# Attention on one Trainium2 core: a second chunk of keys weighted in fp16 halves in place of fp32, its high half split on ScalarE and its low half on GpSimd

## The reference, cut to what matters

```python
q_n, k_n = (rmsnorm(q, g_q), rmsnorm(k, g_k))
scores = scale * np.matmul(q_n, k_n.transpose(0, 1, 3, 2))
scores = scores - np.max(scores, axis=-1, keepdims=True)
attn = np.exp(scores)
attn = attn / (np.sum(attn, axis=-1, keepdims=True) + 1e-09)
return np.matmul(attn, v).astype(np.float32)
```

## Time and profile before

| what | us |
|---|---|
| median of three runs | 1143.07 |
| the profiled execution | 1139.88 |
| its span, first to last instruction | 1138.1 |
| TensorE busy | 1100.3 (97%) |
| VectorE busy | 594.7 (52%) |
| ScalarE busy | 425.9 (37%) |
| GpSimd busy | 256.5 (23%) |
| attention, up to the first matmul of the next layer | 300.5 |
| first scores of step 0 | at 19.4 |
| steps 7 to 21, each | 11.33 |

### The profile page before, as it was taken

How to read it: one execution, slowest core, us unless ns; L and a number is a source line. 1 busy time by engine, 2 the same in 40 slices (tenths; PEclk the granted TensorE clock), 3 DMA queues, 4 the chain that set the end, 5 groups by cost and what they waited for, 6 DMA issues and landing times.

```text
span 1138.1 us, 17823 instructions
## 1 busy us (share of the span) xinstructions
PE 1100.3 (97%) x6617; PEld 573.3 (50%) x6618; DVE 594.7 (52%) x837; ACT 425.9 (37%) x631; POOL 256.5 (23%) x235
## 2 busy tenths in 40 slices
PE   7989999999999999999999999999898999999996
PEld 3434444444455555555555555556454555555554
DVE  7888888887433443333343300015656565556721
ACT  5768777777511111211111200001535253353510
POOL 4756767672200000000000000000211122112211
PEclk9999999999999999999999999999899999999999
DMA  5412222210121111111100501000848355366400
GB/s 144 122 49 62 61 65 58 66 25 17 60 67 56 56 55 55 55 55 55 55 28 1 195 28 41 28 32 23 296 163 319 118 211 206 108 217 225 142 20 18
DMA packets 71978, 104.11 MB, mean 91 GB/s; under 512 B 29310, under 2 KB 47870, under 8 KB 71920
## 3 DMA queue, kind: packets, MB, share of 16 engines
q1 hardware_dynamic: 63680, 89.84, 24.0%
q0 software_dynamic: 3120, 11.02, 2.7%
q10 hardware_dynamic: 5120, 2.48, 0.8%
HBM read 93.88 MB, written 13.76 MB: 95 GB/s over the span
## 4 chain that ended last, share of the span: by engine, by line
PE 87%; ACT 4%; DVE 4%; issue 2%; DMA 2%; ACTq 0%; POOL 0%; DVEq 0%; POOLq 0%; SPq 0%
PE ps L1434 29%; PE ps L1449 15%; PE ps L1528 12%; PE ps L1357 10%; PE ps L1506 7%; PE ps L1336 5%; PE ps L1316 2%; ACT arena L815 2%; DVE arena L1042 2%; PE ps L1348 2%; PE ps L1299 2%; PE ps L1338 1%; DMA arena<-in_moe_w 1%; PE ps L1515 1%; PE ps L1493 1%
## 5 line engine op out<-in xcount | busy, mean ns | idle before, releaser
L1434 PE MATMUL ps<-arena 128*128 128x448 f16 x1728 | 328.8, 352 | 0.0
L1434 PEld LDWEIGHTS ps<-arena 128*128 128x128 f16 x1728 | 168.1, 98 | 155.7
L1449 PE MATMUL ps<-arena 128*128 128x392 f16 (+1 forms) x1008 | 167.3, 329 | 2.4 <-DVE arena L1022 2.4
L1506 PE MATMUL ps<-arena 128*128 128x512 f16 x648 | 150.5, 388 | 5.6 <-DVE arena L1229 5.6
L1042 DVE SCALAR_TENSOR_TENSOR arena<-arena 128x768 f16<-128x768 f32 (+1 forms) x112 | 113.1, 1066 | 74.1 <-ACT arena L815 74.0
L1528 PE MATMUL ps<-arena 128*128 128x384 f16 x864 | 143.3, 326 | 4.0 <-DVE arena L1234 3.6
L1449 PEld LDWEIGHTS ps<-arena 128*128 (+1 forms) x1008 | 98.4, 98 | 70.4 <-DVE arena L1022 2.8
L1357 PE MATMUL ps<-arena 128*128 128x448 f32 x288 | 133.0, 573 | 0.0
L785 ACT ACTIVATE arena<-ps 128x448 f32<-128x448 f32 x48 | 26.1, 543 | 263.0 <-PE ps L1434 263.0
L1016 DVE SCALAR_TENSOR_TENSOR arena<-ps,arena 128x448 f32<-128x448 f32 x48 | 30.0, 624 | 176.0 <-PE ps L1434 96.1
L1528 PEld LDWEIGHTS ps<-arena 128*128 128x128 f16 x864 | 83.5, 98 | 58.6 <-issue 2.5
(11 more groups left out here) (170 smaller groups left out, 1078.7 us busy)
## 6 DMA issues: line engine op xcount, KB each, us to landing
arena<-in_moe_w SPq DMA_DIRECT2D x48, 512.0 KB, 6.3
arena<-in_moe_w SPq DMA_DIRECT2D x64, 384.0 KB, 3.9
arena<-in_qk SPq DMA_DIRECT2D x23, 448.0 KB, 3.5
y_parts<-arena SPq DMA_DIRECT2D x16, 384.0 KB, 2.3
arena<-in_v SPq DMA_DIRECT2D x48, 96.0 KB, 2.6
arena<-in_moe_w_out SPq DMA_DIRECT2D x12, 384.0 KB, 5.5
arena<-in_w_out_t SPq DMA_DIRECT2D x11, 384.0 KB, 3.1
arena<-in_moe_w_gate SPq DMA_DIRECT2D x10, 384.0 KB, 4.2
```

Of the source, the lines that this page charges most:

```text
L1434: last = nc.tensor.matmul(ps[:, 2 * (b % 2) + g, 0:S], up_w[s][:, g, c, wl], xt[:, b * KC + c, xl], start=(c == 0 and wl + xl == 0), stop= ...
L1449: last = nc.tensor.matmul(ps[:, 4 + 2 * s + h, 0:cols], gt[:, f, gl, bass.ds(t * 128, 128)], wo[:, f, wl, h, 0:cols], start=(f == 0 and gl ...
L1506: last = nc.tensor.matmul(ps[:, b, :], x_t[:, xl, c], w1_s[s][:, c, wl, b * 512:(b + 1) * 512], start=(c == 0 and xl + wl == 0), stop=(c = ...
```

## The change

The first of the three chunks of 128 keys is weighted in fp16 halves too. `exps(n, 1)` takes the smaller bias (the factor 256), so that the result fits fp16. ScalarE gets `first_high(n)` (a copy of 128x896 to fp16, after `exps(n, 2)`) and a copy of V's first chunk with its ones (128x192) in `v_high`. VectorE gets the low half of V's chunk in `v_low`, ahead of that of the last keys. GpSimd gets `first_low(n)` (128x896, probabilities less their high half) as the last item of its step. TensorE's `weigh` of chunk 0 becomes `weigh_first`: three fp16 matmuls of 128x448 for each head. There are two buffers of each new tile and four new semaphores; ScalarE also waits at the start until GpSimd has written the ones.

```diff
+        p_first = [at2.take(128, 2 * 2 * S, F16).rearrange("p (l h s) -> p l h s", l=2, h=2) for _ in range(2)]
+        v_first = [at2.take(128, 2 * 3 * D, F16).rearrange("p (l c) -> p l c", l=2) for _ in range(2)]
...
+            def first_low(n):
+
+                pool.wait_ge(p1_hi_ready, n + 1)
+                nc.gpsimd.tensor_tensor(p_first[n % 2][:, 1], probs[n % 2][:, :, 0], p_first[n % 2][:, 0], ALU.subtract)\
+                    .then_inc(p1_lo_ready, 1)
+
             for n in range(3):
                 normalise(n)
...
                 if has(n - 2):
                     x_low(n - 2)
+                if has(n):
+                    first_low(n)
...
-                    nc.scalar.activation(probs[n % 2][:, :, i - 1], ps_pair(SCORE_SLOT, 128), ACT.Exp, bias=lift[:, 1:2])\
+                    nc.scalar.activation(probs[n % 2][:, :, i - 1], ps_pair(SCORE_SLOT, 128), ACT.Exp,
+                                         bias=lift[:, 0:1] if i == 1 else lift[:, 1:2])\
                         .then_inc(probs_ready, 1)
...
+            def first_high(n):
+
+                act.wait_ge(probs_ready, 4 * n + 2)
+                nc.scalar.activation(p_first[n % 2][:, 0], probs[n % 2][:, :, 0], ACT.Copy).then_inc(p1_hi_ready, 1)
+
             def v_high(n):
 
                 act.wait_ge(v_loaded[n % 3], 64 * (n // 3) + 64)
+                nc.scalar.activation(v_first[n % 2][:, 0], v_ones[n % 3][:, 0], ACT.Copy, scale=S_OP).then_inc(v1_hi_ready, 1)
                 nc.scalar.activation(v_parts[n % 2][:, 0], v_end[n % 3], ACT.Copy, scale=S_OP).then_inc(v_hi_ready, 1)
...
             act.wait_ge(lift_ready, 2)
+            act.wait_ge(ones_ready, 3)
             act.wait_ge(scratch_ready, 1)
...
                 if has(n):
                     exps(n, 2)
+                    first_high(n)
                 if has(n - 2):
                     x_high(n - 2)
...
             def v_low(n):
 
+                dve.wait_ge(v1_hi_ready, n + 1)
+                nc.vector.scalar_tensor_tensor(v_first[n % 2][:, 1], v_ones[n % 3][:, 0], S_OP, v_first[n % 2][:, 0], ALU.mult, ALU.subtract)\
+                    .then_inc(v1_lo_ready, 1)
                 dve.wait_ge(v_hi_ready, n + 1)
...
+            def weigh_first(n, h):
+
+                pe.wait_ge(v1_lo_ready, n + 1)
+                pe.wait_ge(p1_lo_ready, n + 1)
+                for pl, vl in PASSES:
+                    nc.tensor.matmul(ps[:, 6 + h, SQ], v_first[n % 2][:, vl, h * D:h * D + 2 * D], p_first[n % 2][:, pl, h],
+                                     start=False, stop=False)
+
             def weigh(n, h, cs):
 
-                if h == 0 and cs[0] == 0:
+                if h == 0:
...
                     weigh_end(n - 1)
-                    weigh(n - 1, 0, (0,))
+                    weigh_first(n - 1, 0)
...
-                    weigh(n - 1, 1, (0,))
+                    weigh_first(n - 1, 1)
```

More of the change, by code:

```diff
@@ L278, in attention_moe_moe_kernel @@
         p_lo_ready = sem("p_lo_ready")
+        p1_hi_ready = sem("p1_hi_ready")
+        p1_lo_ready = sem("p1_lo_ready")
+        v1_hi_ready = sem("v1_hi_ready")
+        v1_lo_ready = sem("v1_lo_ready")
         v_hi_ready = sem("v_hi_ready")
```

## The result

The changed kernel takes 1155.93 us (median of four runs, 1153.12 to 1156.45) against 1142.9 of the kernel before: 1.0111 times the time, 95% interval 1.0089 to 1.0134, that is 13.0 us more. The forecast was 1158.6, in a range of 1148 to 1166, and slower with a chance of 0.87. The profiled execution took 1153.12 us, its span 1151.4, against 1139.88 and 1138.1 before.

What follows compares the result with a forecast made beforehand. TensorE was taken to bound the step, by 0.3 us over ScalarE. Fifteen steady steps at +0.76 us (+11.4) and the uneven steps summed to +15.5: 1143.07 + 15.5 = 1158.6 us, 8 in 10 within 1148 to 1166.

Steps and rivals of the forecast that it cites:

- The mechanism: Each steady attention step: VectorE's low half of V stands some 1.2 us until GpSimd's first_low ends, delaying everything behind it.
- step 4: Uneven attention step: 1.7 us gained as GpSimd's multiplication no longer blocks the low halves, 1.0 lost on ScalarE, -0.7 us together.
- TensorE's saving: Three fp16 passes for each fp32 matmul of the first chunk: up to 0.6 us less TensorE time a step.
- ScalarE's loop: The steady step if ScalarE alone set it, with its two new copies: 11.33 us, no gain, no loss.
- the sum of 12.09 us: Steady step as a loop through ScalarE, GpSimd, VectorE and back to exps: 12.09 us against 11.33, +0.76 a step.
- Step 0: First attention step: scores(1, 0) already waits for ScalarE's exps, so all new ScalarE work shows, +1.1 us.
- Step 6: Attention step with turned_high ahead on ScalarE, no longer covered: +1.1 us.
- Steps 3 and 5: Two attention steps taken to lose like the steady ones: +1.5 us together.
- Steps 1 and 2: Early attention steps, paced by ScalarE's DMA issues: no change, 0 us.
- No blocking: Rival for the steady steps: first_low releases the port early, 0 to 0.1 us a step, 1143 to 1147 us; chance 0.13.
- TensorE's saving comes through: Rival: ScalarE's copies stay hidden in its idle time, 24 x 0.6 = 14 us go, 1129 us; chance 0.05.
- The clock falls in the steady steps: Rival: new TensorE gaps lower the granted clock in each step, 1158.6 + 20 = 1179 us; chance 0.06.

Runs made afterwards that it cites:

- experiments 1: The changed kernel with two neighbours on ScalarE swapped, x_high(n-2) ahead of first_high(n): 1150.65 us against 1144.55 of the kernel before, 1.0054 times.
- experiment 2: The changed kernel without GpSimd's first_low, TensorE's third pass reading the high half again: 1149.58 us against 1144.55 of the kernel before, 1.0041 times.
- experiment 7: The changed kernel with GpSimd's first_low run twice, the second waiting for the first: 1199.93 us in one execution.
- experiment 4: The changed kernel with all four splits left out and the three fp16 passes reading constant tiles: 1134.24 us against 1144.55 of the kernel before, 0.9902 times.
- the repeated profile: The changed kernel run again, nothing altered: 1156.04 us against 1143.46 of the kernel before, 1.0101 times.
- experiment 3: The changed kernel with x_high ahead of first_high and both v_high copies moved behind end_high(n): 1137.94 us against 1144.55 of the kernel before, 0.9945 times.
- experiment 8: The changed kernel with x_high ahead of first_high and a second 128x896 copy behind first_high into a spare tile: 1171.35 us in one execution.

## Why the prediction was right, and where it was off

**The mechanism** of the steady step was right in each link, and shown by experiments 1, 2 and 7: taking the overlap away by order alone, or by leaving the GpSimd instruction out, gives back the same 0.35 us; doubling it adds 1.69. The Trainium skill's page "SBUF — State Buffer", section "SBUF: two separate sides", has the rule that the port pair which the two engines share is held for a whole instruction; the traces agree for the subtractions (1.36 us for L977 in the changed kernel, 1.97 for L984 in experiment 7). The exception seen before the change, the `pow` of 16 columns, stayed one: the two low halves took 0.35 and 0.28 us under it in step 4 of the changed kernel.

**TensorE's saving** was forecast at up to 0.6 us a step and measured alone at 0.55 (experiment 4). **ScalarE's loop** was forecast at 11.33 and measured at 11.40 (experiments 1 and 2). Without GpSimd's part the change is still a loss of some 5 us (experiment 2), but only 1.0 of it lies in steps 7 to 21 (170.95 us against 169.97); the rest is in the uneven ones, where the granted clock fell too (0.77 in step 1, 0.81 in step 4). The saving is eaten at `scores(n+1, 0)`, as written.

**The step that failed** is the size of the loop, the sum of 12.09 us, which measured 11.75. The other links were right to 0.02 us each. Off were:

- `first_low`: 1.89 us and not 2.0. I took a value near twice the 448-column instruction; twice the columns added 0.86 us to its 1.03 and not 1.03 again, and the bounds (1.66 to 2.07) held it.
- `x_low` to the next GpSimd instruction: 1.00 us and not 1.12 (220.99 to 221.99). I had read 1.12 in front of another kind of instruction, the small `tensor_scalar` of `inverse_rms`.
- what is left of the low halves after the release: 0.34 and not 0.45 (223.88 to 224.22).

These 0.34 us times 15 make 5.1 of the 5.2 us between +11.4 and +6.2.

**The uneven parts.** Step 0 came out as worked out: the wait ahead of the next scores grew from 1.06 to 2.15 us. Step 6 came out within 0.1 us; it took 12.87 us with `first_low` left out as well (experiment 2), so GpSimd's part isn't what sets it. Steps 3 and 5 together came out within 0.1 us by luck. Step 3 lost 0.43 us, like a steady step and not the 0.76 of the sum; step 5 lost 1.02, since another VectorE instruction there was held by `first_low`, which I had not seen (the last section shows it; in experiment 2 step 5 is a steady step of 11.40).

In step 4 the low halves of the up weights took 1.83 us and not 3.53, as forecast. The wait for `v_low`, which I had put at 4 us, was 3.61 before and 2.34 now; the step gained 1.22 us, and 2.07 in the repeated profile, where the granted clock stayed at 1.00.

Steps 1 and 2 cost 0.7 us that I had put at nothing, but they gained 0.8 in the repeated profile. Both have the same wait of 2.15 us ahead of step 1 (1.06 before the change); the granted clock in the step is 0.86 in the first and 1.00 in the second. The difference between the two goes with the clock, and the wait alone doesn't explain the clock. I had named the clock as a rival for the steady steps only.

In step 22 and the drain I counted the waits for `first_low` but only one set of the fp16 passes' savings; there are three.

**The whole.** The attention accounts for 9.9 us (10.6 in the repeated profile), the medians say 13.0 and 12.6, with intervals from 10.2 to 15.3 and from 9.3 to 13.7. In the first pair of profiles the rest is in the expert stage, which the change doesn't touch. Its length differs by 7 us between the profiles, and the kernel before alone spreads from 1140.3 to 1147.1 us in 25 runs. The two shortest expert stages are those of the two kernels without the new tiles, which looks like an effect. The medians speak against it: in experiments 1 to 4 the attention differs by +5.4, +5.9, -7.1 and -10.2 us and the medians by +6.1, +5.0, -6.6 and -10.3. And those two profiles are of the shortest executions that their kernels had in these runs, 3.0 and 3.7 us under the medians (1139.88 against 1142.9, 1139.73 against 1143.43). So I count it as chance; that is argued from these figures, and no run was made to show it. My total of +15.5 was thus 5.6 too high for the attention, and by luck came nearer to the median than its working deserved.

**The rivals.** No blocking: fell with the first trace (1.36 us for L977). TensorE's saving comes through: fell for the change as it is; its condition (ScalarE's copies out of the stretch) was met half in experiment 3 and gave 6.6 us. The clock falls in the steady steps: not in this kernel (1.00), but in some steps of experiment 7, which has a gap of 1.40 us ahead of `weigh_end` in every step. A gap's length alone doesn't decide it: the gap of 1.62 us ahead of `scores(n+1, 0)` in experiment 8 left the clock at 1.00.

## What to carry to other kernels

When work moves from a full engine to two that look half idle, lay their instructions on one time line with the third: here it was neither queue's length but the overlap of GpSimd's subtraction with a two-input instruction of VectorE that came first, and swapping two neighbours on a third engine removed it. Then look at the steps that aren't like the others: the same swap put a new overlap of this kind into step 4. Look for the next loop behind the first: a copy that is free in one place of an engine's list (ahead of a wait that is idle anyway) costs its full length in another (between the last two links that TensorE waits for). And test the part that is meant to save by itself, with constant operands: the 0.55 us of experiment 4 said what there was to win, before any order was tried.

## What the runs showed of the hardware that I had not expected

**A VectorE instruction with one SBUF input can be held up too.** In step 5 of the changed kernel `tensor_scalar` on 128x96, fp32 to fp16, from SBUF to SBUF, took 1.22 us behind `first_low`; before, it took 0.20 with only the `pow` beside it, and 0.20 again in experiment 2, which has no `first_low`. The changed kernel, then the kernel before:

```profile
79.27 1.89 POOL L577 TENSOR_TENSOR arena<-arena 128x896 f16<-128x896 f32 x1
...
80.01 1.22 DVE L895 TENSOR_SCALAR arena<-arena 128x96 f16<-128x96 f32 x1
```

```profile
79.55 0.20 DVE L872 TENSOR_SCALAR arena<-arena 128x96 f16<-128x96 f32 x1
```

The reciprocal, one fp32 input as well, and GpSimd's multiplication of 112x1024 did not hold each other up: in the steady step before the change the reciprocal took 2.95 us from 205.19 and the multiplication 1.90 from 206.25, and so did the two in step 4 after it, from 68.89 and 69.27. There the VectorE instruction had started first. In the steady steps of the changed kernel the reciprocal lies over the `pow` and takes 2.94. What sets it apart from the `tensor_scalar` isn't shown here.

**VectorE gets its turn between two GpSimd instructions.** In experiment 7 the gap between the subtractions, 0.08 us, was enough for the low half that stood waiting: it ran from 228.01 to 229.37, into the second subtraction, and the second subtraction was not visibly longer (1.89 us).

**The same gap may or may not cost the clock.** In the drain TensorE waits 1.89 us for `v_low` in both profiles of the changed kernel. In the first the passes behind it run at full speed:

```profile
305.23 0.74 PE L1374 MATMUL ps<-arena 64*128 64x448 f16 x6 [1.89 <-DVE arena L980]
```

In the repeated one the three fp16 passes that follow take 1.29 us and not 0.74, and the drain 1.7 us longer:

```profile
304.24 0.74 PE L1374 MATMUL ps<-arena 64*128 64x448 f16 x6 [1.89 <-DVE arena L980]
...
304.91 1.29 PE L1382 MATMUL ps<-arena 128*128 128x448 f16 x3
```
